# Spreading the next unit's decay preparation over the tiles of a linear-attention stage, and reading the low half of z first

## What is computed

```python
# stage 1: gated linear attention, B, H, S, D = 4, 8, 768, 48
scale = min(|a|, 0.999) / (|a| + 1e-6);  a_n = a * scale          # a = a_re + i a_im
for t in range(S):
    S_re, S_im = (a_n[t] * S).re + k[t] v[t]^T, (a_n[t] * S).im
    y[t] = q[t] @ S_re
# stage 2: x = y as (B*S, H*D) = (3072, 384)
h = x @ w_in                                                     # 384 -> 1024
solu = h * softmax(h);  ln = (solu - mean) / sqrt(var + 1e-6) * g_ln
x2 = ln @ w_out                                                  # 1024 -> 384
# stage 3: top-2 gating on x2 over 8 experts, relu(x2 @ w1[e]) @ w2[e], weighted sum
```

## Time and profile before

| | us |
|---|---|
| median of three runs | 1364.16 |
| lowest and highest run | 1352.96, 1370.98 |
| profiled execution, its own time | 1354.94 |
| its span in the trace | 1353.2 |
| preparation and first tile, to the first `xl` | 116.8 |
| first `xl` to the last `xl` (24 tiles) | 614.2 |
| the rest: last outputs, slot tables, experts | 622.2 |
| TensorE busy, VectorE busy, ScalarE busy, GpSimd busy | 1133.0, 881.1, 620.3, 450.2 |
| granted TensorE clock, mean | 0.93 |

### The profile page before, as it was taken

The page is one execution under the profiler, slowest core; times in us unless marked ns, Lnnn a source line. Parts: engine busy times, 40 slices in busy tenths (PEclk is TensorE's granted clock), DMA queues, the critical chain, the costliest instruction groups (busy, mean ns, idle before and its releaser), DMA issues.

```text
span 1353.2 us, 21866 instructions
## 1 busy us (share of the span) xinstructions
PE 1133.0 (84%) x7864; PEld 981.8 (73%) x7864; DVE 881.1 (65%) x1715; ACT 620.3 (46%) x964; POOL 450.2 (33%) x416
## 2 busy tenths in 40 slices
PE   0017978978978997898999359999999999999996
PEld 0015656655755775576777359999999999999996
DVE  4848658847965875794443357667776667777762
ACT  4331553454445355343443145555555555555551
POOL 3020031224233233221333324444444444444432
PEclk9977988988998997898999669999999999999998
DMA  9220031030122001011111076677767676676650
GB/s 267 93 70 19 22 95 37 25 88 24 32 52 76 25 24 42 24 48 40 28 47 24 7 277 203 222 250 254 240 229 247 238 241 241 234 237 219 227 182 1
DMA packets 85979, 167.50 MB, mean 124 GB/s; under 512 B 18566, under 2 KB 57696, under 8 KB 85872
## 3 DMA queue, kind: packets, MB, share of 16 engines
q1 hardware_dynamic: 72432, 137.71, 32.0%
q0 software_dynamic: 13440, 28.40, 5.9%
HBM read 148.83 MB, written 21.92 MB: 126 GB/s over the span
## 4 chain that ended last, share of the span: by engine, by line
PE 53%; DVE 4%; issue 2%; ACT 2%; DMA 1%; POOL 1%; SPq 0%; POOLq 0%; DVEq 0%; ACTq 0%
PE bank L1301 20%; PE bank L1487 19%; PE bank L1327 4%; PE bank L1363 3%; PE bank L1292 2%; PE bank L1349 2%; PE bank L1402 1%; PE bank L1404 1%; DVE turn L941 1%; PE bank L1431 0%; DVE zl L1104 0%; DVE qp L1026 0%; PE bank L1384 0%; DVE turn L998 0%; DMA mine<-tags 0%
## 5 line engine op out<-in xcount | busy, mean ns | idle before, releaser
L1301 PE MATMUL bank<-sxh,w1h 128*128 128x256 f32 x744 | 212.2, 285 | 1.9 <-DVE sxl L1247 1.9
L854 ACT ACTIVATE hh<-bank 128x256 fp32r<-128x256 f32 x248 | 95.3, 384 | 253.5 <-PE bank L1301 253.5
L1301 PE MATMUL bank<-sxh,w1l 128*128 128x256 f32 x744 | 210.5, 283 | 0.0
L1301 PE MATMUL bank<-sxl,w1h 128*128 128x256 f32 x744 | 210.2, 282 | 0.0
L1270 DVE SCALAR_TENSOR_TENSOR hl<-bank,hh 128x256 fp32r<-128x256 f32 x248 | 104.8, 423 | 117.2 <-ACT hh L854 117.2
L646 POOL DMA_INDIRECT out<-yo,mine x62 | 78.0, 1258 | 273.8 <-DVE yo L1263 264.4
L1487 PE MATMUL bank<-w2h,hh 128*128 128x384 f32 x496 | 167.3, 337 | 0.0
L1487 PE MATMUL bank<-w2l,hh 128*128 128x384 f32 x496 | 166.7, 336 | 0.0
L1487 PE MATMUL bank<-w2h,hl 128*128 128x384 f32 x496 | 166.3, 335 | 0.0
L1301 PEld LDWEIGHTS bank<-sxh,w1h 128*128 128x128 f32 x744 | 140.6, 189 | 2.3 <-DVE sxl L1247 2.3
L1301 PEld LDWEIGHTS bank<-sxh,w1l 128*128 128x128 f32 x744 | 141.7, 190 | 0.0
(11 more groups left out here) (183 smaller groups left out, 2560.7 us busy)
## 6 DMA issues: line engine op xcount, KB each, us to landing
raw<-in_w SPq DMA_DIRECT2D x62, 1536.0 KB, 7.1
ar<-in_a_re SPq DMA_DIRECT2D x6, 768.0 KB, 4.7
turn<-in_a_im SPq DMA_DIRECT2D x6, 768.0 KB, 5.9
qk<-in_q SPq DMA_DIRECT2D x48, 96.0 KB, 2.4
qk<-in_k SPq DMA_DIRECT2D x48, 96.0 KB, 2.5
out<-wide SPq DMA_DIRECT2D x9, 512.0 KB, 11.4
vt<-in_v SPq DMA_DIRECT2D x24, 192.0 KB, 2.7
xs<-x SPq DMA_DIRECT2D x24, 192.0 KB, 2.7
```

The source lines that it names most:

```text
L854: nc.scalar.activation(hh[:, f % NH, :], bank[:, f % 2, 0:CAP], ACT.Relu).then_inc(hh_done, 1)
L1301: ins = MM(dst, stationary[a_](cc), moving[b_](cc), start=(n_ == 0), stop=(n_ == len(terms) - 1))
```

## The change

Five things move; the arithmetic stays the same.

1. VectorE's body begins with the gate copy and `zl`. Before, the group's rank steps, `products_start` and three product operations could stand between them.
2. `norm` moves from the end of body b=0 to body b=1, behind `zl`. The 63 product operations, before 31 by the end of b=1 and 32 in b=2, are now 20, 33 and 10 in b=1, 2, 3. `state_decays` and `f2` go further back in b=3. `newton` stays at the end of b=3.
3. On ScalarE, the first half's `squares` of unit c+2 go to the end of body b=3 of unit c, the second half's behind `zh`, `kt` and `wide` of b=0; `logs` of the first half go ahead of `at`; both `scale`s go behind `xh`; `inverse_squares` go behind the exponential; `inverse` of the second half goes behind `xh`.
4. On GpSimd one `m2` goes to the end of body b=3, ahead of the next unit.
5. In the preparation, unit 1's chain up to `scale` is done ahead of the first tile, and `weights_scaled`, both `weights_rest` and `wo_hi` come behind the first `q_products`. So that this is possible, `raw_in` and `raw_out` no longer share memory with `cum1`.

The core of the diff:

```diff
-        PRODUCTS = {1: 0.5, 2: 1.0}
+        PRODUCTS = (0, 20, 53, 63)
...
+            pool.wait_ge(cum_step, CUM)
+            for q in (2, 3):
+                m2(q)
+            for q in (2, 3):
+                zsum(q)
             pool.wait_ge(w_ready, 2)
...
-                if b == 0 and prep:
-                    m2(2 * c + 2)
+                if b == 0 and prep and c > 0:
                     m2(2 * c + 3)
...
+                if b == 3 and c + 2 < C:
+                    m2(2 * c + 4)
...
-                if b == 0 and prep:
-                    scale(2 * c + 2)
...
                 if b == 3 and prep:
-                    inverse(2 * c + 3)
+                    inverse(2 * c + 2)
                 if has(m):
                     act.wait_ge(y_mm, m + 1)
+                    if m == 0:
+                        act.wait_ge(w_ready, 2)
                     wait(act, h_mm, m)
...
-                if b == 0 and prep:
+                if ahead:
+                    scale(2 * c + 2)
                     scale(2 * c + 3)
+                if b == 3 and prep:
+                    inverse(2 * c + 3)
+                if b == 3 and c + 2 < C:
+                    squares(2 * c + 4)
...
+                if has(j):
+                    dve.wait_ge(zt_hi, j + 1)
+                    wait(dve, x2_mm, j)
+                    V.tensor_tensor(zl[:].rearrange("p c t -> p (c t)"), bank[:, 2:4, :].rearrange("p b x -> p (b x)"),
+                                    zh[:].rearrange("p c t -> p (c t)").bitcast(F32), ALU.subtract).then_inc(zt_lo, 1)
...
+                if b == 1 and prep:
+                    norm(2 * c + 2)
+                    norm(2 * c + 3)
...
+                if b == 1 and prep:
+                    products_start(c + 1)
+                if b == 3 and prep:
+                    state_decays(c + 1)
+                fill(3)
...
                 if n == 0:
+                    weights_scaled()
                     weights_rest(0)
                     weights_rest(1)
                 if b == 3 and prep:
                     newton(2 * c + 2)
                     newton(2 * c + 3)
-                if b == 0 and prep:
-                    norm(2 * c + 2)
-                    norm(2 * c + 3)
```

More of the change, by code:

```diff
@@ L121, in solu_moe_program @@
         cums.append(m1("cum1", [P, 2, NP, 2, BP, HALF, BI]))
+        raw_at = m1.at
         rcs.append(m1("rc1", [P, NP, 2, BP, HALF, BI]))
         z = m1("z", [P, F])
+        zh = m1("zh", [P, FC, P], F32R)
+        zl = m1("zl", [P, FC, P], F32R)
+        xh = m1("xh", [P, NP, P], F32R)
+        xl = m1("xl", [P, NP, P], F32R)
+        x2 = [m1(f"x2_{i}", [P, DM]) for i in range(2)]
+        x2t = m1("x2t", [P, KC, P])
+        assert m1.at >= raw_at + 4 * (NP * F + FC * DM)
         wi_hi = m1("wi_hi", [P, NP, F], F32R)
@@ L144, in solu_moe_program @@
         mds = [m1(f"md{i}", [P, NP, B, 3]) for i in range(2)]
-        xh = m1("xh", [P, NP, P], F32R)
-        xl = m1("xl", [P, NP, P], F32R)
-        zh = m1("zh", [P, FC, P], F32R)
-        zl = m1("zl", [P, FC, P], F32R)
-        x2 = [m1(f"x2_{i}", [P, DM]) for i in range(2)]
-        x2t = m1("x2t", [P, KC, P])
         causal = m1("causal", [P, P])
@@ L717, in _ @@
             nc.scalar.activation(wi_hi[0:PR], raw_in[0:PR], ACT.Copy).then_inc(w_hi_ready, 1)
-            act.wait_ge(w_scaled, FC)
-            nc.scalar.activation(wo_hi[:], raw_out[:], ACT.Copy).then_inc(w_hi_ready, 1)
+            for q in (2, 3):
+                squares(q)
             for q in (0, 1):
@@ L723, in _ @@
                 inverse(q)
+            for q in (2, 3):
+                logs(q)
+            for q in (2, 3):
+                scale(q)
+            act.wait_ge(w_scaled, FC)
+            nc.scalar.activation(wo_hi[:], raw_out[:], ACT.Copy).then_inc(w_hi_ready, 1)
             def body(c, b, n):
@@ L728, in body @@
                 prep = c + 1 < C
[L730 to L738 removed]
+                ahead = b == 0 and prep and c > 0
                 if has(j):
@@ L768, in body @@
                     nc.scalar.activation(spl[:, 1, from_:], spl[:, 0, from_:], ACT.Ln, bias=1.0).then_inc(sp_done, 1)
-                if b == 3 and prep:
-                    inverse_squares(2 * c + 2)
-                    inverse_squares(2 * c + 3)
+                if ahead:
+                    squares(2 * c + 3)
+                    logs(2 * c + 2)
+                if b == 1 and prep:
+                    neg(2 * c + 2)
+                    neg(2 * c + 3)
                 if has(m):
@@ L776, in body @@
                                          bank[:, 2:4, :].rearrange("p b x -> p (b x)"), ACT.Copy).then_inc(a_evac, 1)
-                if b == 0 and prep:
-                    logs(2 * c + 2)
                 if group is not None:
@@ L799, in body @@
                     nc.scalar.activation(x2[par][:], bank[:, 0, 0:DM], ACT.Copy, scale=rstd[par][:, 1:2]).then_inc(x2_evac, 1)
-                if b == 3 and prep:
-                    inverse(2 * c + 2)
                 if has(i):
```

79 lines of the change are left out of this document (34 added, 45 removed).

## The result

The changed kernel takes 1283.3 us (median of four executions, 1276.5 to 1290.96) against 1364.8 before (median of four, 1352.96 to 1370.98): a ratio of 0.9445, with a 95% interval of 0.9353 to 0.9537. The forecast was 1288, the worked sum 1283.6. The profiled execution took 1290.96 (span 1289.2), 64.0 less than that of before, where the sum had 71.3. Between the medians the gain is 81.5. The executions of each kernel lie 14.5 us (after) and 18 us (before) apart, so that the sum and the median agree to 0.3 us is luck. In the profiles three terms of the sum were off, in both directions, and the rest of this text is about them.

A forecast was written before the change was run, and what follows sets the result against it. In the first phase TensorE sets a floor of 23.3 to 24.4 us per body, plus waits for `zl` and clock drops. Gains 47.9 + 3.7 + 19.7 = 71.3 gave 1283.6; adjusted for the median, 1288, range 1271 to 1309.

The forecast's parts named there:

- wait for `zl` into b=0: TensorE's wait from b=3 into b=0: 7.69 less 1.4 (rank steps), 1.6 (GpSimd add), 1.2 (`inverse`) leaves 3.5 us.
- b=0 bodies, four: First body of a unit: floor 23.3, wait 3.5 and clock drop 2.2 give 29.0 us each.
- b=1 bodies: `norm` behind `zl`; TensorE's 5.14 us wait and clock drop go: 24.4 us, between 23.3 and 25.0.
- b=2 bodies: Two more carries between `k_products` and `xl` than before: 24.84 + 0.5 = 25.3 us, ends 24.0 and 26.3.
- b=3 bodies: Ten carries among the gate steps delay the maximum some 2 us, which falls into slack: floor of 24.4 us.
- body 20, gain: Wait of 4.57 loses 2.6 and 2.0 stay; gain 2.6 or 4.8 depending on the clock, taken 3.7 us.
- preparation, gain: Before the units: first `xl` at about 95.3 instead of 116.83, less 1.8 back in b=2: 19.7 us, ends 14 and 23.
- The rival in which the add is the one that stands still: GpSimd's remaining add yields to `newton` before b=0: wait 1.6 shorter, 1282 us; chance 0.17 together with the clock holding.
- The clock's price: TensorE's lower clock after the wait into b=0: 2.2 us per body, up to about 4.9.
- slower* rival: Small waits at hidden-layer starts or `zl` keep TensorE at low clock: bodies of 38 us, six to seven make it slower; chance 0.02.
- VectorE becomes the bound: Bodies b=1 to b=3 each lose 1.7 us more than taken, 20 in all: 1308 us; chance 0.16.
- the low half of z first does nothing: `newton` stays ahead, so the wait into b=0 stays 7.7 with its clock drop: 1307 us; chance 0.08.

The follow-up runs named there:

- the first experiment: Kernel before with only `zl` moved directly behind the gate copy in VectorE's body: 1354.98 us, ratio 1.001.
- the kernel with the squares back: Changed kernel with the first half's `squares` and GpSimd's `m2` moved from the end of b=3 back into b=0: 1265.72 us, ratio 0.9382.
- both edits: Changed kernel with `newton` behind `zl` in the next b=0, and the first half's `squares` and `m2` back in b=0: 1247.85 us, ratio 0.9236.
- the two further ones: Changed kernel, unchanged, run twice more, one execution each: 1294.64 and 1283.46 us.
- made to order: Changed kernel with `newton` behind `zl`, plus four extra VectorE maxima ahead of `zl` in bodies 4, 8, 12 and 16: 1272.79 us, ratio 0.9438.

## Why the forecast was right, and which of its terms were not

By its own terms, in the profiled executions (71.3 forecast, 64.0 measured):

| term | forecast | measured |
|---|---|---|
| wait for `zl` into b=0 | 3.5 | 3.53, three times (4.60 in body 4) |
| b=0 bodies, four | 4 x 29.0 = 116.0 | 134.8 |
| b=1 bodies | 24.4 | 25.3 to 25.7 |
| b=2 bodies | 25.3 | 24.2 |
| b=3 bodies | 24.4 | 22.7 |
| these three kinds, four units | 296.4 | 289.3 |
| four units, gain | 47.9 | 36.2 |
| body 20, gain | 3.7 | 3.5 |
| preparation, gain | 19.7 | 24.6 |

**The wait into b=0** was right, and so were the parts that the experiments take singly: 1.4 for the rank steps (7.68 to 6.30 in the first experiment), 1.6 for one GpSimd add (1.67, shown by putting the add back), 2.0 left in body 20 (1.87). That leaves 1.1 for the `inverse` (1.2 forecast), which no run isolates. The rival in which the add is the one that stands still didn't come, because the add was under way 0.03 us before the `newton` operation that it held (246.33 and 246.36). In the opposite order it is the add that waits: in body 4 of the kernel with the squares back it starts at 148.92, 0.08 behind a `newton` operation, and takes 2.55 where it takes 1.83 alone, while that operation keeps its 0.96. The Trainium skill, page "SBUF — State Buffer", section "Who interferes with whom", says that the port which the two engines share is an exclusive lock and that the order of issue decides who is blocked; both orders agree with it. What the prediction didn't see is behind these 3.5: ScalarE's two squares ahead of `zh` hold another 0.76 that shows only when `newton` is gone. They cost nothing while `newton` is the later of the two.

**The clock's price** is the step that failed. The prediction put 2.2 us behind every such wait, with 4.9 as its upper end, "so b=0 is 23.3 + 3.5 + 2.2 = 29.0". The floor was right (23.8 with both edits), and where the clock recovered, so was the sum: 28.49 and 29.57. But in bodies 8 and 16 the clock stayed down for 27.3 us, nearly to the end of the body, and they took 38.4 each: 11 us for the clock behind a wait of 3.53. Together the b=0 bodies are 18.8 us longer than forecast. With the floors of the kernel with both edits (93.6 for four) and the waits (15.2), the clock took 25.9 where 8.8 was forecast: 17.1 of the 18.8. Body 4's longer wait is another 1.2, the floor 0.4. The rows of before could have warned only in part: they held drops of 2.2 and 4.9 behind longer waits, and no body of 38 us. The prediction had that figure all the same: the *slower* rival worked out 38 us for a body at the low clock, and gave it a chance of 0.02. It was the right number at another place, `zl` into b=0 instead of the hidden layer's start, and in two places instead of the six that it needed.

**The other bodies** were 7.1 us better in sum. The rival *VectorE becomes the bound* (1308) is wrong with the new dealing of the products. With the old one TensorE does wait for VectorE, and the kernel measured 1304 even with `newton` out of the way; 19 operations instead of 8 then stand between `k_products` and `xl` in b=1. Where it erred is the floor of 24.4 for a b=3 body, which it took from scores to scores; from `xl` to `xl` such a body takes 22.7, and b=1, with the most matmuls (186), takes 25.3. The sum over a unit hardly changes with the cut: 94.3 forecast as four floors, 94.6 measured with both edits in the first of the four units and 96.0 to 96.4 in the others. In these, TensorE's waits behind `xl` in b=1 and b=2 are 2.3 to 2.7 together, where the forecast had put 3.1 on top of the floors of these two bodies. The rest of the 7.1 comes from where a body is cut.

**The preparation** gave 4.9 more than forecast. The first `xl` was 1.9 earlier, and the 1.8 us "back" in the b=2 body that follows didn't come: it took 23.15, 1.15 less than the 24.30 before. The b=3 body behind it is unchanged (24.33, and 24.35 before). Here the parts agree with an experiment only in part: on the kernel before, the early start alone moved `xl` to 97.57; the other 4 us belong to the dealing of the products (97.39 when the old dealing is put back).

**Body 20** gained 3.5 in this execution, in which the clock held. In one of the two further ones it took 29.83, more than the 28.86 before.

**Sum.** 64.0 is 71.3 less 18.8 for the b=0 bodies and 0.2 for body 20, plus 7.1 and 4.9, within 0.3. The forecast held because errors of 19 and 12 us opposed each other, which is luck. The rival *the low half of z first does nothing* was right for that edit alone on the kernel before (ratio 1.001), and wrong within the change. The changed kernel wasn't as good as its parts: `newton` behind `zl` and the first add and squares back in b=0 give 1247.9, another 35 us.

**What stays open** is why the clock stays down for 27 us of dense work after one wait of 3.53 and for 3 after the next. The length of the wait doesn't tell them apart: bodies of 38 us came behind 3.53 here and behind 4.4 in the first experiment, and none behind the 7.69 of before or the 3.30 made to order in the profiled executions. The moment of the fall does, among the nine bodies with a wait of 3.53, but it is no rule for other waits: in body 16 of the kernel with the made wait the clock fell 0.26 us before the scores and was back after 10.2, and in the two long bodies of the first experiment it fell 0.6 after their start. What brings it back wasn't tested.

## What to carry to other kernels

Where TensorE works densely, price a wait not by its length alone but by its length and what the clock does behind it: here waits of 0.76 us cost themselves, and waits of 1.9 to 3.5 cost one to four times themselves, with a spread from one execution to the next. So it pays to bring the last short waits to nothing, and a change that shortens nearly every wait can gain nothing, as the first experiment did. Before an operation is moved ahead of a released one, read all three lists at that place (here `newton` on VectorE, an add on GpSimd, the squares or the negation on ScalarE): only the latest of them shows as a wait, and the next one is found when it is gone.

## What the runs showed of the hardware that was not expected

- The same wait in the same body of the same program ends in bodies of 29.38 or 38.34 us, at a mean granted clock of 0.88 or 0.64; 176 matmuls keep TensorE busy for 25 us or for 35. A wait of 1.87 (body 20) was followed by the lower clock once in three traces of the changed kernel (29.83 instead of 25.3), and one of 1.86 or 1.87 in three bodies of four with the squares back.
- With waits up to 0.76 us the granted clock stayed at 1.00 in bodies 8, 12 and 16 of three kernels (24.36 to 24.39 us): `newton` behind, and this with `norm` back or with the old dealing.
- A GpSimd add of 768 columns (1.83 us) beside a VectorE operation of the same size on two SBUF inputs: the one that starts second takes longer by about what is left of the first, and the first keeps its time. VectorE took 2.62 instead of 0.95 when it started 0.03 us behind the add, and the add 2.55 instead of 1.83 when it started 0.08 behind VectorE. So less than 0.1 us in the start decides which engine pays.
